# Moving the scatters of attention's rows to the middle of TensorE's products with V, one iteration sooner

## What is computed

```python
# attention: 8 heads of 64, each query sees its own and the 63 keys before it
scores = (q @ k.T) / 8;  scores = where(0 <= i - j < 64, scores, -1e9)
x = softmax(scores) @ v                        # -> [2304, 512]
# mixture of experts: 8 experts, 512 -> 1024 -> 512, each row goes to its two best
noisy = x @ w_gate + log1p(exp(x @ w_noise)) * noise
top2 = two largest of noisy;  gate = softmax(noisy[top2])
y = sum over the two e of gate_e * (relu(x @ w1[e]) @ w2[e])
# feed forward: 512 -> 2048 -> 512
h = y @ w_in;  out = (h * clip(h + 3, 0, 6) / 6) @ w_out
```

## Time and profile before

| | |
|---|---|
| median of three runs | 1028.59 us |
| the profiled execution's own time | 1034.54 us |
| its span | 1032.8 us |
| TensorE busy (products) | 1004.4 us, 97% |
| TensorE busy (weight loads) | 891.6 us, 86% |
| VectorE, ScalarE, GpSimd busy | 413.7, 230.7, 428.0 us |
| share of the chain that ended last | PE 93%, DVE 2%, issue 2%, DMA 1%, ACT 1% |
| scatters (L682) | 36, 35.7 us in all |

### The profile page before, as it was taken

One profiled execution on the slowest core, in us unless ns is written; L12 is line 12 of the kernel. 1 busy time (PEld: TensorE's weight loads), 2 busy tenths in 40 slices (PEclk: granted clock), 3 DMA queues, 4 the chain that ended last, 5 costly groups with the idle time before them and its releaser, 6 DMA issues.

```text
span 1032.8 us, 19975 instructions
## 1 busy us (share of the span) xinstructions
PE 1004.4 (97%) x8116; PEld 891.6 (86%) x8116; DVE 413.7 (40%) x879; ACT 230.7 (22%) x537; POOL 428.0 (41%) x335
## 2 busy tenths in 40 slices
PE   7989879999999999999999999999999999999998
PEld 6767668999989899999989988999999999999997
DVE  2566564322222131222222146535445445354433
ACT  3665541211111111111111112111111111111111
POOL 3566755996482909375482937300101001000000
PEclk8999989999999999999999999999999999999999
DMA  7797468866261715336241444110101011100000
GB/s 174 186 225 200 133 202 288 262 188 214 83 221 47 218 67 176 141 107 210 83 165 55 131 130 164 41 53 21 41 30 41 20 42 40 41 1 1 31 1 31
DMA packets 106795, 116.25 MB, mean 113 GB/s; under 512 B 27616, under 2 KB 74208, under 8 KB 106720
## 3 DMA queue, kind: packets, MB, share of 16 engines
q1 hardware_dynamic: 88672, 75.36, 25.7%
q10 hardware_dynamic: 12288, 20.98, 5.8%
q0 software_dynamic: 5760, 18.88, 5.5%
HBM read 76.13 MB, written 39.06 MB: 112 GB/s over the span
## 4 chain that ended last, share of the span: by engine, by line
PE 93%; DVE 2%; issue 2%; DMA 1%; ACT 1%; SPq 0%; ACTq 0%; DVEq 0%
PE PS L1576 22%; PE PS L1560 22%; PE PS L1696 19%; PE PS L1680 19%; PE PS L1365 2%; PE PS L1445 2%; PE PS L1544 2%; PE PS L1424 1%; PE PS L1408 1%; DMA k_raw<-in_k_dram 1%; PE PS L1621 1%; PE PS L1457 1%; PE PS L1386 1%; DMA x_in<-x_sorted 0%; PE PS L1477 0%
## 5 line engine op out<-in xcount | busy, mean ns | idle before, releaser
L1576 PE MATMUL PS<-W,hs_room 128*128 128x512 f32 x960 | 245.6, 399 | 0.0
L1560 PE MATMUL PS<-xs,W 128*128 128x256 f32 (+1 forms) x1536 | 242.3, 308 | 0.3 <-issue 0.3
L1560 PEld LDWEIGHTS PS<-xs,W 128*128 128x128 f32 x1536 | 232.9, 188 | 10.8 <-issue 0.7
L1696 PE MATMUL PS<-W,gs 128*128 128x512 f32 x864 | 217.0, 395 | 0.9 <-DVE gs L1294 0.9
L1680 PE MATMUL PS<-x2s,W 128*128 128x384 f32 x1152 | 216.6, 337 | 0.0
L1680 PEld LDWEIGHTS PS<-x2s,W 128*128 128x128 f32 x1152 | 201.2, 188 | 7.3
L654 POOL TENSOR_TENSOR W<-stage,ones_f 128x1024 fp32r<-128x1024 f32 (+1 forms) x100 | 147.3, 1484 | 142.1 <-PE PS L1576 137.4
L1576 PEld LDWEIGHTS PS<-W,hs_room 128*128 128x128 f32 x960 | 174.6, 188 | 33.4 <-DVE hs_room L1145 0.2
L1696 PEld LDWEIGHTS PS<-W,gs 128*128 128x128 f32 x864 | 161.2, 188 | 31.8 <-issue 1.6
L662 POOL TENSOR_TENSOR W<-stage,W 128x1024 fp32r<-128x1024 f32 (+1 forms) x100 | 185.4, 1865 | 5.8
L1145 DVE SCALAR_TENSOR_TENSOR hs_room<-PS,hs_room 128x256 fp32r<-128x256 f32 (+1 forms) x128 | 62.8, 491 | 293.7 <-ACT hs_room L858 291.3
(11 more groups left out here) (135 smaller groups left out, 592.5 us busy)
## 6 DMA issues: line engine op xcount, KB each, us to landing
stage<-in_moe_w_dram SPq DMA_DIRECT2D x64, 512.0 KB, 4.5
y_sorted<-y_sb ACTq DMA_DIRECT2D x40, 256.0 KB, 2.9
x_in<-x_sorted ACTq DMA_DIRECT2D x38, 256.0 KB, 4.7
x_sorted<-zeros SPq DMA_DIRECT2D x7, 1280.0 KB, 7.7
vD<-in_v_dram SPq DMA_DIRECT2D x72, 64.0 KB
out_dram<-o_sb SPq DMA_DIRECT2D x18, 256.0 KB, 2.0
stage<-in_moe_w_in_dram SPq DMA_DIRECT2D x8, 512.0 KB, 4.4
stage<-in_moe_w_out_dram SPq DMA_DIRECT2D x8, 512.0 KB, 3.6
```

Source lines behind the costliest of these rows:

```text
L1560: last = nc.tensor.matmul(HP_[:, c % 2, 0:n], W[:, par, 0, b, at:at + P], xs[part][:, a, kd, :], start=start, stop=(kd == KD - 1 and (a, b ...
L1576: last = nc.tensor.matmul(Y[:, first + t, :], hs[:, c % 2, a, t * P:(t + 1) * P], W[:, par, 1, b, c * DM:(c + 1) * DM], start=(c == 0 and ...
L1696: last = nc.tensor.matmul(OP[:, tt, :], gs[:, c % 2, a, tt * P:(tt + 1) * P], W[:, 1, c // FC, b, at:at + DM], start=(c == 0 and (a, b) == ...
```

## The change

The table of scatters now begins at iteration 7 instead of 8 and reaches to 17 instead of 15, so that tiles 0 to 9 have an iteration each, all but iteration 10 and one tile sooner than before. TensorE raises a new semaphore, `v_half`, when half of a tile's products with V are done. The first scatter of a tile in the table (k = 0) waits for `v_half` of the iteration that the table names. The second follows after two of the four high pieces, or after a pause. The trailing loop now holds tile 10 alone.

```diff
-    SCATTER_AT = {8: 0, 9: 1, 10: 2, 12: 3, 13: 4, 14: 5, 15: 6}
+
+    SCATTER_AT = {7: 0, 8: 1, 9: 2, 11: 3, 12: 4, 13: 5, 14: 6, 15: 7, 16: 8, 17: 9}
...
+        v_half = sem("v_half")
...
-            def split_hi(parity, c, pieces=1):
+            def split_hi(parity, c, pieces=1, first=0, end=None):
+
                 n = CH // pieces
-                for at in (slice(i * n, (i + 1) * n) for i in range(pieces)):
+                for at in (slice(i * n, (i + 1) * n) for i in range(first, pieces if end is None else end)):
...
-                last.then_inc(w_half, 1)
+                if end is None:
+                    last.then_inc(w_half, 1)
...
+                if k == 0 and t in SCATTER_AT.values():
+                    pool.wait_ge(v_half, min(T for T in SCATTER_AT if SCATTER_AT[T] == t))
                 pool.indirect_dma_start(out=x_sorted,
...
             for T in range(2, max(SCATTER_AT) + 1):
                 keep_x(T - 2)
+                if T in SPLIT_AT:
+                    first_there(SPLIT_AT.index(T))
                 if T in SCATTER_AT:
                     scatter(SCATTER_AT[T], 0)
-                if T in SPLIT_AT:
-                    first_there(SPLIT_AT.index(T))
-                    split_hi(0, SPLIT_AT.index(T), PIECES)
-                elif T in SCATTER_AT:
-                    pause()
-                if T in SCATTER_AT:
+                    if T in SPLIT_AT:
+                        split_hi(0, SPLIT_AT.index(T), PIECES, 0, PIECES // 2)
+                    else:
+                        pause()
                     scatter(SCATTER_AT[T], 1)
                 if T in SPLIT_AT:
+                    split_hi(0, SPLIT_AT.index(T), PIECES, PIECES // 2 if T in SCATTER_AT else 0)
                     split_lo(0, SPLIT_AT.index(T), SPLIT_AT.index(T) + 1, PIECES)
 
-            for t in range(LOTS[FIRST_LOT][0], LOTS[FIRST_LOT + 1][0]):
+            for t in range(max(SCATTER_AT.values()) + 1, LOTS[FIRST_LOT + 1][0]):
                 for k in range(2):
                     pause()
                     scatter(t, k)
-            for t in range(max(SCATTER_AT) - 1, TILES - 1):
+            for t in range(max(SCATTER_AT) - 1, TILES):
                 keep_x(t)
-            keep_x(TILES - 1)
...
+                    if hp == HP // 2 - 1:
+                        last.then_inc(v_half, 1)
                 last.then_inc(out_full, 1)
```

## The result

The kernel with the change takes 1032.98 us (median of 7 runs, 1030.90 to 1034.91), the kernel before 1029.57 us (7 runs, 1028.06 to 1031.23). The ratio is 1.0039, 95% interval 1.0024 to 1.0054: slower by 4.0 us (2.5 to 5.6). The profiled execution took 1033.59 us, its span is 1031.8 us; that of before had 1034.54 and 1032.8. So the two profiled executions stand in the other order than the medians, and comparing them needs care.

The account below looks back on a forecast made before the run. TensorE (97% busy) was taken as the bound, with expert 0's start and clock deciding. Loads +0.3, block turns +0.5 and expert clock +0.5 gave +1.3 us on the 1028.59 us median: 1029.9 us, range 1024.5 to 1034.0.

Parts of the forecast that it names:

- (a): Attention iterations 8 to 14: first scatters of pairs hidden, second ones still costing 0.58 us each; -3.5 us.
- (b): Attention iteration 15: turned q and k no longer late, but routing steps slowed by GpSimd's low pieces; +0.2 us.
- (c): Attention iteration 16: four scatters become two; -1.0 us, bounds 0 and -2.7.
- (d): Attention iteration 17: TensorE's clock fall expected to shrink, products and transposes quicker; -1.6 us.
- g: Time by which tile 16's products with V, the last but one, come sooner; summed to 5.9 us.
- (e): Attention's end: four scatters and three pauses behind tile 16's half products delay expert 0's loads by 6.2 - g; +0.3 us.
- (f): From loads to expert 0: TensorE idles, then turns the blocks at half clock; +0.5 us.
- (g): Expert 0's start: low clock may reach into its products; +0.5 us, bounds 0 and 3.4.
- R1: Rival, faster: attention gains about 11 us, more than the scatter queue takes; 1024.6 us, chance 0.22.
- R2: Rival, slower: scatters cost TensorE nothing, attention gains 1 us, loads leave 5.2 us later; 1034.8 us, chance 0.10.
- R3: Rival, slower: the clock stays low for a long stretch within expert 0; 1032.8 us, chance 0.17.
- R4: Rival, slower: GpSimd runs late, so first scatters fall into scores and turning; 1031.7 us, chance 0.09.

Follow-up runs that it names:

- e1: The kernel before, unchanged, run and profiled again on the first chip; 1027.15 us, ratio 0.9993 to the kernel before.
- e12: The kernel before with shorter pauses (256 columns copied instead of 512) between its last scatters, third chip; ratio 0.9997.
- e9: The change, unedited, run again on the third chip; ratio 1.0049 to the kernel before.
- e10: The change for tiles 0 to 6, tiles 7 to 10 scattered in a paused train as in the kernel before, third chip; ratio 1.0018.
- e11: e10 with the train's pauses copying 256 columns instead of 512, third chip; ratio 1.0007 to the kernel before.
- e6: The change with tile 7 moved to iteration 16 and tile 8 to 17, so six scatters follow the last release, second chip; ratio 1.0056.
- e7: The kernel before without the pauses between attention's eight last scatters, second chip; ratio 1.0054.
- e5: Same kernel as e10, run on the second chip; ratio 0.9990 to the kernel before.
- e3: The change with tile 9's scatters moved to the end of iteration 16 and tile 10's pair put in iteration 17; ratio 1.0034.
- e2: The change plus 24 unused products of zeros on TensorE ahead of expert 0's first turned block; ratio 1.0025.
- e4: e3 plus twelve unused products of zeros on TensorE; ratio 1.0047 to the kernel before.

## Why the prediction came out as it did

The forecast was +1.3 us with a range of -4.1 to +5.4; measured +3.4 between the medians, 4.0 by the ratio. It was slower, which had 0.42, and the range held it. That the range held it is partly luck: the queue was priced right, but of the 5.9 us that were set against it 0.7 were there in e1's terms (5.2 too much), and two smaller errors, the wait that the kernel before has already (1.6) and the clock (about 1), ran the other way.

- **(a), -3.5 us for hidden first scatters: the step that failed.** Twelve scatters at 0.58 us were read from one profiled execution. In e1 and e12 (placement of before), the change, e9, e10 and e11 (the new one) there is no such price: 44.3 us from tile 6 to tile 13 with the placement of before, 44.6 to 44.8 with the new one. The prediction saw the warning, that this execution was 6 us above the median, and passed over it: "the sum is a difference within it and I put it on the median". The 7.0 us of holes are about those 6 us. What they cost in that execution, the timed runs did not pay, so the change could not give it back. (The undisturbed 44.7 was near the truth by luck: e1's stretch is six iterations of 6.05 us and one with routing of 7.99, not six of 6.3 and one of 6.9.) On the second chip the stretch behaves as the step says, 52.5 against 48.7, -3.8; the timed runs there cannot confirm it.
- **(b), (c), (d).** Iteration 15 took 8.06 (change) and 8.09 us (e1), 8.28 in the profile that was priced: -0.2 or 0.0 for +0.2 forecast. The fall of the clock came as expected, at 120.8, and is in both (117.7 in e1). Iteration 16 took 6.59 instead of 7.60, -1.0 as forecast in number; but e12, with the placement of before in these iterations, takes 14.1 for the two where e1 takes 15.7 and the change 14.65, so this is not shown to be the change's. Iteration 17 took 4.49 in both, no gain for -1.6: its clock was full in e1 too.
- **g.** Forecast 5.9. It is 11.0 against the profile that I read, and 0.7 against e1, which the timed runs resemble. Neither is 5.9: (a) had taken the middle of a term that is either there or not.
- **(e), the step that decides: right, with one term missing.** Half of tile 16's products to the loads, four scatters and three pauses: 9.2 us behind tile 16's products (9.1 forecast). But "loads later by 6.2 - g" took the loads of before to leave with ScalarE's last copy, 2.9 us behind tile 16. When attention is undisturbed, the train of before is what they wait for, 4.5 us behind. So the loads leave 9.17 - 4.54 - 0.70 = 3.9 us later than in e1. The first two of these numbers are waits behind tile 16's products in the two profiles; the sum splits the measured delay and is no test of it. The tests are e6 and e10.
- **(f), (g), +1.0 for the clock.** From the loads to the second dozen it takes 12.8 us with the change and 11.8 in e9, 12.4 in e1 and 10.6 in the first profile. Against the profile that was priced this stretch is 2.2 us longer for +1.0 forecast; against e1 it is +0.3 and -0.7, nothing that can be told, and the half-speed dozen is there in both kernels. The length of the wait does not decide it either: TensorE waited 7.96 us for the loads in e6, more than the change's 6.39, turned the blocks at half clock and had expert 0's first dozen at full clock (2.32 us). The section of the Trainium skill that the prediction named ("TensorE: Matmul & The Clock Gate", "Loop structure matters more than you think") does describe what TensorE did in the change: cold behind the wait for the loads. What it does not give is a difference between these kernels, since before waits too.
- **R1** had the g of the first profile and needed it in the timed runs. **R2**, that scatters cost TensorE nothing, is near what happened on quiet chips, with g = 0.7 for 1, and had a chance of only 0.10; its 1034.8 was too high because it lacked the wait that the kernel before has already, and by its clock. The Trainium skill's rule that stood beside it ("SBUF — State Buffer", "SBUF: two separate sides") agrees with e1 and with the change. As a rule on time it fails in e7, where ScalarE and VectorE stood idle under eight scatters and TensorE got its products in handfuls; both engines are marked there as waiting for a signal ("<-remote"), and nothing shows a port as the cause. **R3**'s mechanism happened, in e1 as in the change. **R4**'s lateness is real for three of seven: the first scatters of iterations 9, 13 and 14 started 3.1, 3.0 and 5.2 us behind their half of the products, and cost nothing.

What stays open is what puts an execution into the one state or the other. All four profiles on the second chip had the holes, the eight on the first and third and the change's own had none of over 0.2 us from tile 6 to the end of attention, and the first profile of before had them though none of its kernel's seven timed runs came near its 1034.54 us. That speaks for the chip, and is no proof.

## What to carry to other kernels

Before you price a term from a profiled execution, see whether its own time lies among the timed runs; where it is 6 us above them and you find 7 us of unexplained holes, these are likely the same microseconds, and a change that removes them gains nothing in the timed runs. Work that is spread along a stage by a signal per iteration has its last pieces behind the last signal: count what stands there and its rate, and set it against when an unpaced queue would have been done, which may already be what the next stage waits for. And where two engines could hold the same wait, take out both before you write a formula with one.

## What had not been expected of the hardware

- Scatters with addresses from the chip disturb the other engines in some executions and not in others, with the same program: holes of 0.15 to 0.42 us in dense products, iterations without routing of 6.5 to 9.0 us instead of 6.05 to 6.25, and medians of the kernel before of 1035.1 against 1028.0 and 1028.6 us.
- In that state eight unbroken scatters (1.28 us apart) kept VectorE idle for 11.87 and ScalarE for 9.65 us; with the starts 1.78 us apart (e5, same chip) VectorE's longest wait in the train was 3.35 and ScalarE's 2.29 us, each ended by TensorE. During expert 0 rows of scatters 1.28 us apart held nobody, in e7 as well.
- From the start of the last scatter to its landing it took 2.7 to 2.8 us in the change, e1, e3, e6 and e9, but 3.2 to 4.1 in e2, e4, e11 and e12, which takes back part of what a train that ends sooner gives.
- 5.5 us of products of zeros moved the fall of the clock from 141.2 to 146.3 us, and expert 0's first dozen was at 1.2 GHz all the same (4.18 us in e2 and in the change); a bridge over a part of the wait did not help the dense work behind it.
